# f_logit loaded in 32x32 blocks and turned by VectorE in place of TensorE's transposes

## What is computed

```python
f = 1.0 / (1.0 + np.exp(-f_logit))
for t in range(S):                      # attention
    state = f[:, :, t, :, None] * state + einsum('bhd,bhde', k[:, :, t], v[:, :, t])
    y[:, :, t] = einsum('bhd,bhde->bhe', q[:, :, t], state)
x = y.transpose(0, 2, 1, 3).reshape(B * S, H * D)
h = x @ w_in                            # first layer, 384 -> 2048 -> 384
x = (h * sigmoid(1.702 * h)) @ w_out
for e in range(4):                      # second layer, 4 experts, 384 -> 1024 -> 384
    out += p[:, e:e+1] * (relu(x @ w1[e]) @ w2[e])
```

## Time and profile before

| | us |
|---|---|
| median of 3 runs (1537.58 to 1538.17) | 1537.62 |
| span of the profiled execution, first to last instruction | 1534.4 |
| PE busy in the span | 1492.8 (97%) |
| DVE, ACT, POOL busy | 631.7, 441.9, 426.7 |
| mean granted clock of PE, of 1 | 0.994 |

### The profile page before, as it was taken

The page is one execution under the profiler, slowest core; times in us unless marked ns, Lnnn a source line. Parts: engine busy times, 40 slices in busy tenths (PEclk is TensorE's granted clock), DMA queues, the critical chain, the costliest instruction groups (busy, mean ns, idle before and its releaser), DMA issues.

```text
span 1534.4 us, 24075 instructions
## 1 busy us (share of the span) xinstructions
PE 1492.8 (97%) x8824; PEld 1409.7 (92%) x8824; DVE 631.7 (41%) x951; ACT 441.9 (29%) x793; POOL 426.7 (28%) x390
## 2 busy tenths in 40 slices
PE   7799999999999999999999999999999999999999
PEld 6799999999989999999999999999999999999998
DVE  8773634537363553722343233232223223323323
ACT  6442434334242434424322111111111111111111
POOL 7554444435354444535300100100100100000000
PEclk9799999999999999999999999999999999999999
DMA  8620402222040221001311001010010010100011
GB/s 157 147 33 1 76 4 48 32 47 32 2 79 1 47 32 32 1 23 55 114 46 42 0 0 41 0 41 1 0 41 0 0 41 0 41 0 0 21 41 62
DMA packets 125675, 52.99 MB, mean 35 GB/s; under 512 B 104096, under 2 KB 120992, under 8 KB 125600
## 3 DMA queue, kind: packets, MB, share of 16 engines
q1 hardware_dynamic: 125600, 51.96, 14.8%
HBM read 42.52 MB, written 9.44 MB: 34 GB/s over the span
## 4 chain that ended last, share of the span: by engine, by line
PE 86%; DVE 5%; issue 4%; POOL 3%; ACT 1%; DMA 0%; DVEq 0%; SPq 0%; POOLq 0%; ACTq 0%
PE bank L959 12%; PE bank L958 12%; PE bank L957 12%; PE bank L1140 9%; PE bank L1138 9%; PE bank L1139 9%; PE bank L1002 7%; PE bank L1085 4%; PE bank L1086 3%; PE bank L1087 3%; PE bank L1036 3%; DVE scores_T L819 2%; PE bank L978 1%; POOL decays L466 1%; PE bank L1033 1%
## 5 line engine op out<-in xcount | busy, mean ns | idle before, releaser
L720 ACT ACTIVATE h_h<-bank 128x512 fp32r<-128x512 f32 x192 | 114.8, 598 | 637.0 <-PE bank L959 637.0
L1140 PE MATMUL bank<-we_h,h_l 128*128 128x384 f32 x768 | 257.2, 335 | 0.0
L1138 PE MATMUL bank<-we_h,h_h 128*128 128x384 f32 x768 | 257.0, 335 | 0.0
L1139 PE MATMUL bank<-we_l,h_h 128*128 128x384 f32 x768 | 256.9, 334 | 0.0
L911 DVE SCALAR_TENSOR_TENSOR h_l<-bank,h_h 128x512 fp32r<-128x512 f32 x192 | 132.7, 691 | 284.3 <-ACT h_h L720 284.3
L557 POOL TENSOR_TENSOR we_l<-we_raw,we_h (+1 forms) x48 | 63.1, 1315 | 621.7 <-ACT we_h L710 621.7
L541 POOL TENSOR_TENSOR g_l<-sig,g_h 128x384 fp32r<-128x384 f32 x128 | 155.1, 1212 | 289.0 <-ACT g_h L665 289.0
L959 PE MATMUL bank<-x,we_l 128*128 (+1 forms) x576 | 225.0, 391 | 0.0
L958 PE MATMUL bank<-x,we_h 128*128 (+1 forms) x576 | 224.9, 391 | 0.0
L957 PE MATMUL bank<-x,we_h 128*128 (+1 forms) x576 | 224.0, 389 | 0.0
L922 DVE SCALAR_TENSOR_TENSOR acc<-bank,p_n,acc 128x384 f32 (+1 forms) x192 | 105.2, 610 | 266.1 <-PE bank L1140 266.1
(11 more groups left out here) (92 smaller groups left out, 2080.3 us busy)
## 6 DMA issues: line engine op xcount, KB each, us to landing
we_raw<-in_moe_w SPq DMA_DIRECT2D x16, 768.0 KB, 6.0
f_raw<-in_f_logit SPq DMA_DIRECT2D x24, 192.0 KB, 4.6
q_raw<-in_q SPq DMA_DIRECT2D x24, 192.0 KB, 4.6
k_raw<-in_k SPq DMA_DIRECT2D x24, 192.0 KB, 5.1
v_sb<-in_v SPq DMA_DIRECT2D x24, 192.0 KB, 4.1
x_dram<-work SPq DMA_DIRECT2D x8, 576.0 KB, 3.5
x_raw<-x_dram SPq DMA_DIRECT2D x12, 384.0 KB, 4.0
out_dram<-acc SPq DMA_DIRECT2D x5, 768.0 KB, 3.5
```

The costliest lines, as they stand in the source:

```text
L1138: pe.matmul(dst, hh, wh, start=j == 0, stop=False)
L1139: pe.matmul(dst, hh, wl, start=False, stop=False)
L1140: last = pe.matmul(dst, hl, wh, start=False, stop=j == GT - 1)
```

## The change

From half 1 on the gate is not transposed by PE any more. f_logit is loaded already cut into blocks: 16 DMAs for a half, one for each pair of heads and each quadrant of 32 partitions. A quadrant takes the first 32 or the other 16 of a head's 48 dimensions; a partition holds one of every 32 steps. ACT applies the sigmoid in place to the 128 x 1536 elements of `f_raw`, DVE turns all the 32 x 32 blocks in one instruction into `gate_T` (same layout as before), and a semaphore `gate_ready` tells POOL, DVE and SP. Half 0 keeps PE's transposes, in banks of their own. The ring has 3 units less for each half.

```diff
@@ SP
+                sp.wait_ge(gate_ready, n * CH)
+                for r in range(PAIRS):
+                    for i in range(QUADS):
+                        lo = SQ * (i % 2)
+                        width = min(SQ, D - lo)
+                        sp.dma_start(f_blocks[i * SQ:(i + 1) * SQ, r, :, 0:width],
+                                     f_blocks_v[b, a, 2 * r + i // 2, :, :, lo:lo + width]).then_inc(f_blocks_loaded, 16)
...
@@ POOL, step q, ahead of next_decay(n, 0)
-                    pool.wait_ge(read_by["act"], n * PER_HALF["act"] + CH)
+                    pool.wait_ge(gate_ready, (n + 1) * CH)
...
@@ ACT, step gate
+                    if c == "gate" and not fine(n):
+
+                        act.wait_ge(f_blocks_loaded, n * 16 * F_LOADS)
+                        act.activation(f_blocks, f_blocks, ACT.Sigmoid).then_inc(gate_sigmoid, 1)
...
@@ DVE
+                if s == "transpose" and c == "gate" and not fine(n):
+
+                    dve.wait_ge(gate_sigmoid, n)
+
+                    dve.wait_ge(kg_ready, ((n - 1) * LEVELS + 1) * CH)
+                    dve.wait_ge(decay_ready, (n - 1) * LEVELS + 1)
+                    dve.transpose(gate_T[:, :].rearrange("p (r t x) -> p r t x", r=PAIRS, x=SQ), f_blocks)\
+                        .then_inc(gate_ready, CH)
...
-                        dve.wait_ge(read_by["act"], n * PER_HALF["act"] + 2 * CH)
+                        dve.wait_ge(gate_ready, (n + 1) * CH)
+                        dve.wait_ge(read_by["act"], n * PER_HALF["act"] + CH)
                         dve.tensor_tensor(q_T[:, :], q_T[:, :], gate_T[:, :], ALU.mult).then_inc(qf_ready, CH)
...
@@ PE
+                    if c == "gate":
+                        if not fine(n):
+                            return
```

More of the change, by code:

```diff
@@ L186, in moe_of_attention_kernel @@
     units, level_unit, chunk_unit = [], {}, {}
-    for name in ("gate", "q", "k"):
+    for name in ("q", "k"):
         for i in range(CH):
@@ L240, in moe_of_attention_kernel @@
         q_loaded, k_loaded, f_loaded = ([sem(f"{n}_loaded{c}") for c in range(CH)] for n in ("q", "k", "f"))
-        v_loaded = sem("v_loaded")
+        v_loaded, f_blocks_loaded = sem("v_loaded"), sem("f_blocks_loaded")
+        gate_turned, gate_sigmoid, gate_ready = (sem(n) for n in ("gate_turned", "gate_sigmoid", "gate_ready"))
         pads_zero, pool_built, zeros_ready = sem("pads_zero"), sem("pool_built"), sem("zeros_ready")
@@ L595, in step @@
                 if s == "transpose":
[L596 to L599, removed]
+                    if c == "gate" and not fine(n):
+                        act.wait_ge(f_blocks_loaded, n * 16 * F_LOADS)
+                        act.activation(f_blocks, f_blocks, ACT.Sigmoid).then_inc(gate_sigmoid, 1)
+                    if c == "gate" and fine(n):
+                        for i in range(CH):
+                            act.wait_ge(gate_turned, i + 1)
+                            act.activation(gate_T[:, :].rearrange("p (r i m) -> p r i m", r=PAIRS, i=CH)[:, :, i, :],
+                                           gate_bank[i][:, :].rearrange("p (r m) -> p r m", r=PAIRS),
+                                           ACT.Sigmoid).then_inc(gate_ready, 1)
+                    for i in range(CH if c == "q" else 0):
+                        u = i
                         act.wait_ge(unit_ready, n * UNITS + u + 1)
-                        dst = gate_T if c == "gate" else q_T
-                        act.activation(dst[:, :].rearrange("p (r i m) -> p r i m", r=PAIRS, i=CH)[:, :, i, :],
+                        act.activation(q_T[:, :].rearrange("p (r i m) -> p r i m", r=PAIRS, i=CH)[:, :, i, :],
                                        ring[u % 3][:, :].rearrange("p (r m) -> p r m", r=PAIRS),
-                                       ACT.Sigmoid if c == "gate" else ACT.Copy).then_inc(read_by["act"], 1)
+                                       ACT.Copy).then_inc(read_by["act"], 1)
                 if s == "level":
@@ L963, in step @@
                 if s == "transpose":
-                    raw, loaded, first = {"gate": (f_raw, f_loaded, 0), "q": (q_raw, q_loaded, CH),
-                                          "k": (k_raw, k_loaded, 2 * CH)}[c]
-                    if isinstance(n, int) and n == 0 and c == "gate":
+                    if c == "gate":
+                        if not fine(n):
+                            return
                         pe.wait_ge(pads_zero, 3)
                         pe.wait_ge(pool_built, 3)
+                        for i in range(CH):
+                            pe.wait_ge(f_loaded[i], 16)
+                            for r in range(PAIRS):
+                                pair = f_raw[:, i * H + 2 * r:i * H + 2 * r + 2, :].rearrange("p j x -> p (j x)")
+                                last = pe.transpose(gate_bank[i][:, r * P:(r + 1) * P], pair, ident[:, :])
+                            last.then_inc(gate_turned, 1)
+                        return
+                    raw, loaded, first = {"q": (q_raw, q_loaded, 0), "k": (k_raw, k_loaded, CH)}[c]
                     for i in range(CH):
```

21 lines of the change are left out of this document (14 added, 7 removed).

## The result

| | before | after |
|---|---|---|
| median of 4 runs, us | 1537.82 (1537.58 to 1538.17) | 1558.32 (1556.86 to 1560.43) |
| span of the profiled execution | 1534.4 | 1558.7 |
| PE busy | 1492.8 (97%) | 1497.5 (96%) |
| PE instructions | 8824 | 8740 |
| mean granted clock of PE | 0.994 | 0.985 |

The changed kernel is slower: 1.0136 times the time of before, 95% interval 1.0124 to 1.0148, or 20.5 us between the medians. The forecast was 1551.8, the range 1543 to 1564. The profiled execution of after is the longest of its four (their spans are 1555.1 to 1558.7), so the two traces differ by 24.3 us. What follows accounts for those 24.3. The mean granted clock of the other three executions is 0.984 to 0.987; 50 to 40 us at half rate would give that, by an estimate from their spans, so this part of the loss differs from one execution to the next.

A forecast was written before the change was run, and what follows sets the result against it. The prediction took PE, busy for 97% of the span, as the bound, with POOL's list as second runner. It added 10.2 us for the later gate and 4 us for PE's lower clock to 1537.6, giving 1551.8, range 1543 to 1564.

The follow-up runs named there:

- the late diagonal products: DVE's diagonal products moved from slot 4 to slot 10: kernel before 1525.02 us, changed kernel 1544.34, changed kernel with gate turned in the previous pass's last slot 1516.23.
- three DMAs: Changed kernel with each half of f_logit loaded by 3 DMAs as before the change, in place of 16, so the logits are wrongly placed: 1558.15 us.
- half a transpose: Changed kernel with DVE transposing only 768 of the gate's 1536 columns, the rest of gate_T left from an earlier half: 1551.86 us.

## What to carry to other kernels

Read a gap of the bound engine in one piece and not by its sum: 3.7 us at one place cost 1.6 us of lateness in a pass and 1.4 us or more in clock, and waits of 1 to 2 us at two places of a pass cost no clock. To move work to an idle engine, look first at who reads the result and how long before the reader the work could stand; here the same transposes cost 19 us in slot 0 and gained 9 one slot earlier (both with the late diagonal products). Where an engine's queue has work without a deadline (the diagonal products) ahead of work that the bound engine waits for, exchange them.

## What the runs showed of the chip

- The granted clock of PE fell to 0.50 with 27 of the 31 single gaps of 2.17 to 3.67 us that the thirteen traces have in the dense work of the passes, and with none of the many of 1.38 to 1.74. The twelve of 3.51 and 3.67 all brought it. Below that the length alone doesn't settle it: gaps of 2.96 and 2.94 us in half 5 of two kernels (three DMAs; the changed one with the late diagonal), and of 3.07 and 2.29 in half 1 of the changed kernel and of the one with half a transpose, left the clock at 1.00, while one of 3.06 in half 1 of the changed kernel with the late diagonal did not.
- Where half 0 goes over into half 1 PE has one or two waits of 1.2 to 2.1 us close together, and there low clock of 3.4 us (once 6.8) stands in twelve of the thirteen traces.
- At the 27 gaps the low stretch lasted 3.4 us, or 6.8, and began between 1.6 us ahead of the gap's end and 1.5 us behind it. The six that lasted 6.8 all began before the gap ended, by 0.63 to 1.59 us; of the 3.4 us ones none began more than 0.56 us before it. It appears in no list of waits: only in windows, in a first matmul of 0.68 us in place of 0.44, or in matmuls that start 0.32 us apart and not 0.17. Whether the early start is the cause of the 6.8 no run tests.
- Adding 24 matmuls per pass into the gap made a kernel 9.3 us faster.
- The transpose of 128 x 1536 in fp32 took 1.77 us on VectorE, and that of 128 x 768 0.97: 1.04 ns for each element more in a row.
